# Transposing the hidden rows between an expert's two layers with VectorE's 32 by 32 blocks and a trip through memory

## The reference, cut to what matters

```python
for e in range(E):                                   # E = 8
    for k in range(2):
        mask = top2[:, k] == e
        h = np.maximum(x[mask] @ w1[e], 0.0)         # [n, 512] @ [512, 1024], ReLU
        out[mask] += top2_w[mask, k, None] * (h @ w2[e])   # [n, 1024] @ [1024, 512]
```

## Time and profile before

| what | value |
|---|---|
| median of 3 runs | 1077.09 us (1076.47 to 1077.72) |
| the profiled execution | 1075.87 us, its span 1074.0 us |
| granted TensorE clock | 0.999 of full speed |
| TensorE busy | 1062.9 us, 99% |
| VectorE busy | 586.2 us, 55% |
| ScalarE busy | 328.3 us, 31% |
| GpSimd busy | 386.9 us, 36% |
| experts' stage | from about 560 us to the end |

### The profile page before, as it was taken

The page is one execution under the profiler, slowest core; times in us unless marked ns, Lnnn a source line. Parts: engine busy times, 40 slices in busy tenths (PEclk is TensorE's granted clock), DMA queues, the critical chain, the costliest instruction groups (busy, mean ns, idle before and its releaser), DMA issues.

```text
span 1074.0 us, 20103 instructions
## 1 busy us (share of the span) xinstructions
PE 1062.9 (99%) x6053; PEld 932.2 (87%) x6054; DVE 586.2 (55%) x1226; ACT 328.3 (31%) x724; POOL 386.9 (36%) x358
## 2 busy tenths in 40 slices
PE   8999999999999999999999999999999999999997
PEld 7888999999999999999988888888888888888886
DVE  6887344363463463453447775555565555556553
ACT  7986222342432432432352111020303020110231
POOL 4667990030030030210184424060706042240586
PEclk9999999999999999999999999999999999999999
DMA  8985525411311312211175435271626244332676
GB/s 230 283 269 183 161 88 190 125 60 30 118 60 30 117 59 34 93 60 30 47 238 166 140 97 158 44 207 41 195 49 173 71 131 118 88 92 49 171 243 222
DMA packets 199635, 133.18 MB, mean 124 GB/s; under 512 B 128753, under 2 KB 161409, under 8 KB 199585
## 3 DMA queue, kind: packets, MB, share of 16 engines
q1 hardware_dynamic: 177728, 75.14, 25.9%
q10 hardware_dynamic: 16032, 38.47, 11.1%
q0 software_dynamic: 5824, 18.95, 5.1%
HBM read 85.87 MB, written 42.73 MB: 120 GB/s over the span
## 4 chain that ended last, share of the span: by engine, by line
PE 97%; DVE 1%; ACT 1%; issue 1%; DMA 0%; DVEq 0%; SPq 0%; ACTq 0%
PE bank L872 28%; PE bank L1040 22%; PE bank L1061 22%; PE bank L904 14%; PE bank L1074 3%; PE bank L816 2%; PE bank L843 2%; PE bank L826 1%; PE bank L810 1%; PE bank L957 1%; DMA k_sb<-in_kT 0%; ACT p_sb L1216 0%; PE bank L1139 0%; PE bank L885 0%; DVE xT L1234 0%
## 5 line engine op out<-in xcount | busy, mean ns | idle before, releaser
L872 PE MATMUL bank<-x_parts,mlp_weights 128*128 128x384 f32 x1704 | 309.4, 336 | 0.0
L872 PEld LDWEIGHTS bank<-x_parts,mlp_weights 128*128 128x128 f32 x1704 | 298.3, 188 | 5.3
L1040 PE MATMUL bank<-expert_parts,xT_high 128*128 (+1 forms) x688 | 216.7, 396 | 0.0
L1061 PE MATMUL bank<-expert_parts,hT_high 128*128 (+1 forms) x688 | 212.3, 390 | 1.4 <-DVE hT_low L1818 1.4
L731 POOL TENSOR_TENSOR expert_parts<-raw_expert_a,expert_parts 128x512 fp32r<-128x512 f32 x64 | 81.4, 1306 | 234.2 <-ACT expert_parts L1366 231.9
L904 PE MATMUL bank<-mlp_weights,hidden_parts 128*128 128x512 f32 x648 | 162.2, 395 | 0.0
L1061 PEld LDWEIGHTS bank<-expert_parts,hT_high 128*128 128x128 f32 x688 | 129.1, 188 | 28.6 <-issue 2.0
L1040 PEld LDWEIGHTS bank<-expert_parts,xT_high 128*128 128x128 f32 x688 | 125.8, 188 | 24.3 <-issue 0.4
L904 PEld LDWEIGHTS bank<-mlp_weights,hidden_parts 128*128 128x128 f32 x648 | 120.3, 188 | 23.3 <-issue 1.0
L1040 PE MATMUL bank<-expert_parts,xT_low 128*128 (+1 forms) x344 | 134.5, 391 | 0.0
L1061 PE MATMUL bank<-expert_parts,hT_low 128*128 (+1 forms) x344 | 134.3, 390 | 0.0
(11 more groups left out here) (220 smaller groups left out, 1229.6 us busy)
## 6 DMA issues: line engine op xcount, KB each, us to landing
raw_expert_a<-in_w ACTq DMA_DIRECT2D x32, 512.0 KB, 4.6
raw_expert_b<-in_w ACTq DMA_DIRECT2D x32, 512.0 KB, 4.0
x_row<-routed_rows SPq DMA_DIRECT2D x172, 64.0 KB, 2.6
expert_rows<-y_row SPq DMA_DIRECT2D x43, 256.0 KB, 2.0
expert_rows<-zeros SPq DMA_DIRECT2D x4, 2304.0 KB, 11.8
v_sb<-in_v SPq DMA_DIRECT2D x32, 256.0 KB, 4.0
q_sb<-in_qT SPq DMA_DIRECT2D x15, 288.0 KB, 3.7
k_sb<-in_kT SPq DMA_DIRECT2D x15, 288.0 KB, 4.3
```

The lines of the kernel that those rows point to most:

```text
L872: last = nc.tensor.matmul(bank[:, 0:CHUNK], w_sb[:, i, wp, at:at + P], xp[:, par, part, k, :], start=n == 0, stop=n == 3 * KB - 1)
L1040: last = nc.tensor.matmul(ps[half][:, 0:512], (xTh, xTl)[xp][:, buf, k, :], ew_sb[:, bass.ds(slot, 1), wp, k * F2 + half * 512:k * F2 + ha ...
L1061: last = nc.tensor.matmul(y_bank(t)[:, 0:D], (hTh, hTl)[hp][:, f, :], ew_sb[:, bass.ds(slot, 1), 2 + wp, f * D:(f + 1) * D].rearrange("p a ...
```

## The change

For tiles 4 to 41 TensorE no longer transposes the hidden rows. VectorE transposes the 32 by 32 blocks of each half on the way out of PSUM into a new buffer `hB`, without the ReLU (`dve_turn`). SyncE stores `hB` (512 KB) to a scratch tensor in memory, waits for it, and loads it back in four DMAs, one for each quarter of the partitions, into `relu`, so that each block is in its transposed place (`move_hidden`). VectorE then takes the ReLU and splits into `hTh` and `hTl`: per half one `tensor_scalar` and four `scalar_tensor_tensor` of 128 columns (`dve_hidden`). Tiles 0 to 3 and 42 go through TensorE as before; the last tile is reordered, with its transposes between the two halves of the second layer of tile 41, and its result goes to bank 4.

```diff
--- before.py
+++ after.py
@@ -55,6 +55,7 @@
     xT_dram = nc.dram_tensor("xT_scratch", [PAIRS, P, TOKENS], F32).ap()
     xs_dram = nc.dram_tensor("routed_rows", [E * STRIDE, D], F32).ap()
     ye_dram = nc.dram_tensor("expert_rows", [ETILES * P, D], F32).ap()
+    hs_dram = nc.dram_tensor("hidden_by_blocks", [P, F2], F32).ap()
 
 
     ROW = 512
@@ -90,6 +91,9 @@
     raw_mlp = at("raw_mlp", [P, 2, COLS], F32, STAGE_OFF)
     raw_exp_a = at("raw_expert_a", [P, 2, 1024], F32, STAGE_OFF)
     y_sb = at("y_sb", [P, CHUNK_TILES, D], F32, STAGE_OFF + 2 * 4096)
+
+    hB = at("hidden_blocks", [P, F2], F32, STAGE_OFF + 2 * 4096)
+    assert F2 <= CHUNK_TILES * D
 
     yT_sb = at("yT_sb", [P, CHUNK_TILES, KB, P], F32, STAGE_OFF + D * 4)
     assert D * 4 + CHUNK_TILES * KB * P * 4 <= 2 * 4096
@@ -346,7 +350,10 @@
         hTh_done = sem("hTh_done")
         hTl_done = sem("hTl_done")
         tile_done = sem("tile_done")
-        second_tile_half_done = sem("second_tile_half_done")
+
+        half_done = sem("half_done")
+        hidden_out = sem("hidden_out")
+        hidden_in = sem("hidden_in")
         y_row_done = sem("y_row_done")
         y_row_out = sem("y_row_out")
         ye_zeroed = sem("ye_zeroed")
@@ -402,6 +409,9 @@
 
 
 
+        FIRST_TURNED = 4
+
+
         TO_T, TO_PV = 3, 4
 
 
@@ -587,12 +597,31 @@
             load_rows(3, 1)
             load_rows(4, 0)
             store_rows(1)
-            with sp.Fori(0, (ETILES - 5) // 2) as m:
+            load_rows(5, 1)
+            store_rows(2)
+            load_rows(6, 0)
+
+            def move_hidden(t):
+
+                sp.wait_ge(relu_done, 2 * t + 2)
+                sp.dma_start(hs_dram, hB[:]).then_inc(hidden_out, 16)
+                sp.wait_ge(hidden_out, 16 * (t + 1 - FIRST_TURNED))
+                blocks = hs_dram.rearrange("(s r) (h q n) -> q r h s n", s=BLOCKS, h=2, q=BLOCKS)
+                for q in range(BLOCKS):
+                    sp.dma_start(relu[q * BLOCK:(q + 1) * BLOCK, :].rearrange("r (h s n) -> r h s n", h=2, s=BLOCKS),
+                                 blocks[q]).then_inc(hidden_in, 16)
+
+            assert FIRST_TURNED == 4 and (ETILES - 3 - FIRST_TURNED) % 2 == 0
+            with sp.Fori(0, (ETILES - 3 - FIRST_TURNED) // 2) as m:
                 for a in range(2):
-                    load_rows(2 * m + (5 + a), (5 + a) % 2)
-                    store_rows(2 * m + (2 + a))
-            for t in range(ETILES - 3, ETILES):
-                store_rows(t)
+                    move_hidden(2 * m + (FIRST_TURNED + a))
+                    load_rows(2 * m + (FIRST_TURNED + 3 + a), (FIRST_TURNED + 3 + a) % 2)
+                    store_rows(2 * m + (FIRST_TURNED - 1 + a))
+            for t in range(ETILES - 3, ETILES - 1):
+                move_hidden(t)
+                store_rows(t - 1)
+            store_rows(ETILES - 2)
+            store_rows(ETILES - 1)
 
             sp.wait_ge(y_row_out, 16 * ONE + 16 * ETILES)
             sp.wait_ge(rows_out, 16 * (CHUNKS - 1 + CHUNK_TILES))
@@ -1045,12 +1074,12 @@
 
         def y_bank(t):
 
-            return ps[4] if isinstance(t, int) and t == 2 else ps[5]
+            return ps[4] if isinstance(t, int) and t in (2, ETILES - 1) else ps[5]
 
         def pe_down2(pe, t, slot, expert, halves=(0, 1)):
             if halves[0] == 0:
                 pe.wait_ge(expert_low, 16 * expert + 16)
-                if not (isinstance(t, int) and t in (0, 2)):
+                if not (isinstance(t, int) and t in (0, 2, ETILES - 1)):
 
                     pe.wait_ge(y_row_done, ONE + t)
             n = 3 * 4 * halves[0]
@@ -1062,7 +1091,7 @@
                                                 ew_sb[:, bass.ds(slot, 1), 2 + wp, f * D:(f + 1) * D].rearrange("p a n -> p (a n)"),
                                                 start=n == 0, stop=n == 3 * FB2 - 1)
                         n += 1
-            last.then_inc(tile_done if halves[-1] == 1 else second_tile_half_done, 1)
+            last.then_inc(tile_done if halves[-1] == 1 else half_done, 1)
 
         def pe_hT(pe, t):
             for b in range(2):
@@ -1111,10 +1140,8 @@
 
                 now = entries(t)
                 before = entries(t - 1)
-                pe_hT(pe, t - 1)
                 pe_up2(pe, t, buf, *now)
                 pe_down2(pe, t - 1, *before)
-                return now
             fourth = entries(3)
             pe_up2(pe, 3, 1, *fourth)
             fifth = entries(4)
@@ -1125,10 +1152,15 @@
             with pe.Fori(0, (ETILES - 7) // 2) as m:
                 tile(2 * m + 5, 1)
                 tile(2 * m + 6, 0)
-            tile(ETILES - 2, (ETILES - 2) % 2)
-            now = tile(ETILES - 1, (ETILES - 1) % 2)
-            pe_hT(pe, ETILES - 1)
-            pe_down2(pe, ETILES - 1, *now)
+            t = ETILES - 1
+            tile(t - 1, (t - 1) % 2)
+            now = entries(t)
+            before = entries(t - 1)
+            pe_up2(pe, t, t % 2, *now)
+            pe_down2(pe, t - 1, *before, (0,))
+            pe_hT(pe, t)
+            pe_down2(pe, t - 1, *before, (1,))
+            pe_down2(pe, t, *now)
 
         @block.tensor
         def _(pe):
@@ -1806,9 +1838,9 @@
 
         def dve_hT(dve, t, halves=(0, 1)):
             for b in halves:
-                dve.wait_ge(hT_done, 2 * t + b + 1)
-                if isinstance(t, int) and t == 2 and b == 0:
-                    dve.wait_ge(second_tile_half_done, 1)
+                dve.wait_ge(hT_done, 2 * min(t, FIRST_TURNED) + b + 1)
+                if isinstance(t, int) and t in (2, ETILES - 1) and b == 0:
+                    dve.wait_ge(half_done, 1 if t == 2 else 2)
                 elif not (isinstance(t, int) and t == 0):
 
                     dve.wait_ge(tile_done, t)
@@ -1822,11 +1854,38 @@
         def dve_relu(dve, t, halves=(0, 1)):
             for half in halves:
                 dve.wait_ge(up_done, 2 * t + half + 1)
-                if not (isinstance(t, int) and t == 0):
+                if isinstance(t, int) and 0 < t < FIRST_TURNED:
 
                     dve.wait_ge(hT_done, 2 * t - 1 + half)
+                elif isinstance(t, int) and t == ETILES - 1:
+
+                    dve.wait_ge(hTl_done, 2 * t)
                 nc.vector.tensor_scalar(relu[:, half * 512:half * 512 + 512], ps[half][:], 0.0, None, ALU.max
                                         ).then_inc(relu_done, 1)
+
+        def dve_turn(dve, t):
+
+            for half in range(2):
+                dve.wait_ge(up_done, 2 * t + half + 1)
+                nc.vector.transpose(hB[:, half * 512:half * 512 + 512].rearrange("p (q f c) -> p q f c", q=BLOCKS, c=BLOCK),
+                                    ps[half][:].rearrange("p (f q c) -> p q f c", q=BLOCKS, c=BLOCK)
+                                    ).then_inc(relu_done, 1)
+
+        def dve_hidden(dve, t):
+
+            dve.wait_ge(hidden_in, 16 * BLOCKS * (t + 1 - FIRST_TURNED))
+            dve.wait_ge(tile_done, t)
+            for b in range(2):
+                landed = relu[:, b * 512:b * 512 + 512].rearrange("p (s f c) -> p f s c", s=BLOCKS, c=BLOCK)
+                h = hTh[:, 4 * b:4 * b + 4, :].rearrange("p f (s c) -> p f s c", c=BLOCK)
+                nc.vector.tensor_scalar(h, landed, 0.0, None, ALU.max).then_inc(hTh_done, 1)
+                dve.wait_ge(hTh_done, 2 * t + b + 1)
+                low = hTl[:, 4 * b:4 * b + 4, :].rearrange("p f (s c) -> p f s c", c=BLOCK)
+                for s in range(BLOCKS):
+                    last = nc.vector.scalar_tensor_tensor(out=low[:, :, s], in0=landed[:, :, s], scalar=0.0,
+                                                          in1=h[:, :, s].bitcast(F32), op0=ALU.max,
+                                                          op1=ALU.subtract)
+                last.then_inc(hTl_done, 1)
 
         def dve_y(dve, t):
             dve.wait_ge(tile_done, t + 1)
@@ -1863,25 +1922,29 @@
             dve_xT(dve, 4, 0, 2)
             dve_relu(dve, 3)
             for t, extra in ((4, dve_places), (5, dve_combine)):
-                dve_hT(dve, t - 1)
-                dve_relu(dve, t)
+                if t == FIRST_TURNED:
+                    dve_hT(dve, t - 1)
+                else:
+                    dve_hidden(dve, t - 1)
+                dve_turn(dve, t)
                 dve_xT(dve, t + 1, (t + 1) % 2, (t + 1) // 2)
                 extra(dve, link)
                 dve_y(dve, t - 1)
 
             def tile(t, buf, earlier):
-                dve_hT(dve, t - 1)
-                dve_relu(dve, t)
+                dve_hidden(dve, t - 1)
+                dve_turn(dve, t)
                 dve_xT(dve, t + 1, buf, earlier)
                 dve_y(dve, t - 1)
             with dve.Fori(0, (ETILES - 7) // 2) as m:
                 tile(2 * m + 6, 1, m + 3)
                 tile(2 * m + 7, 0, m + 4)
             t = ETILES - 1
-            dve_hT(dve, t - 1)
+            dve_hidden(dve, t - 1)
             dve_relu(dve, t)
+            dve_hT(dve, t, (0,))
```

(2 more changed lines are left out.)

## The result

The changed kernel takes 1173.07 us (median of 4 runs, 1169.91 to 1175.42) against 1077.40 for the kernel before on the same chip: ratio 1.088, 95% interval 1.087 to 1.090. It is slower by 95.7 us. The profiled execution took 1169.91 us, its span is 1168.1.

The account below looks back on a forecast made before the run. TensorE alone was taken to set the 11.80 us tile, with an 11.9 us loop through memory and VectorE in its place; -2.3 + 5 + 65 + 12.5 = +80 on 1075.87 gave 1156 us, range 1072 to 1195.

Parts of the forecast that it names:

- rival A: Experts' stage: hidden-row loop is about 11.9 us and GpSimd takes turns with VectorE; 1156 us, own range 1120 to 1190; 46%.
- Quiet tiles: Tiles without expert weight loading: trip through memory and VectorE takes 11.9 us against 11.8 before, about +5 over 38 tiles.
- Rival D: Short loop hidden behind TensorE's 10.9 us, and VectorE keeps the port shared with GpSimd; 1067 us, down to 1041; 15%.
- Turns with GpSimd: In six weight-loading bursts, VectorE's short two-input instructions of hidden(t) wait for GpSimd's subtractions: 8.8 us a burst.
- the case that I priced at 2.5 and left out: VectorE's SBUF-to-SBUF copies in hidden(t) are blocked by GpSimd too: 2.5 us more, not counted in the sum.
- Rival B: Loop about 11.9 us, but VectorE keeps the port over its four short instructions, waiting once a half; 1111 us; 22%.
- Transfers in a burst: Stores and loads of hidden rows land later beside the expert weight loads: 2.0 us in each of six bursts.
- the first trip's loads meet one weight piece: A burst's first hidden-row loads meet just one weight piece; a full meeting was put at 1.4 us for loads.
- the next, delayed, what is left of them: A burst's second hidden-row trip comes late and meets only the remaining weight loads; both trips together 2.0 us a burst.
- The end: Last five tiles: the trip is slowed beside the gathers and GpSimd's adds, 2.5 us each, 12.5 in all.
- The last tile: Reordered tile 42: TensorE's hole of 2.27 us, waiting for VectorE to split the transposed halves, goes; -2.3 us.
- SyncE's queue: The x rows and y store standing behind the waiting move are issued within 9.7 us, under 11.9: costs nothing.

## Why the prediction was right

Right: the sign, the size (1156 for 1173, within 1072 to 1195) and the mechanism, rival A. That the sum came within 14 us of its execution (1169.91) is in part luck, as its terms were off in both directions: quiet tiles came 16 us cheaper than forecast, bursts 18 dearer, the end 8 and the last tile 4.

- **Quiet tiles.** 11.9 was predicted, 11.46 measured. The store took 2.57 (2.9 in the sum), the three issue steps 1.95 (1.65; within the 1.2 to 2.2), the last landing 3.06 (2.5, and above its upper bound of 2.9), hidden(t) 2.54 (3.1, below its lower bound of 2.6), the turn 1.31 (1.33), and the gaps between engines 0.1 (0.44). What made hidden(t) short: 512 columns are copied from SBUF to SBUF in 0.43 us, 1.5 times the pace of line 1196 in the earlier trace rows. That is the Trainium skill's rule (VectorE: DVE Perf Modes, Mode 2×_2P), by which such a copy runs twice as fast; the trace agrees with it (from SBUF to PSUM the same columns take 0.69). The row is read rightly, but it doesn't stand for this copy; no run shows why line 1196 is slower. The Trainium skill's 2.0 us and bytes over 436 GB/s (DMA: Bandwidth & Descriptors, Anatomy of one DMA) made an estimate of 3.2 for the store, and the trace has 2.57; the section measured DMAs that GpSimd issues, and this one is SyncE's. In all -12.6 + 1.7 = -11 in place of +5: the loop is a little shorter than TensorE's old tile, and longer than its new one. Rival D asked for 10.9.
- **Turns with GpSimd.** 8.8 a burst was predicted with the copies not blocked; 10.3 read and 10.4 measured alone. The four short instructions of a half wait about as the step said (5.05 and 5.09 in place of 0.90 each, 8.3 more); the copies are blocked too, another 1.28 + 1.50 - 0.85 = 1.9. That is the case that I priced at 2.5 and left out. Rival B falls: VectorE does not keep the port between its instructions.
- **Transfers in a burst.** 2.0 was predicted; 13.9 - 10.3 = 3.6 is paid on top of the turns, and 6.8 to 8.3 without them. The term was too small in both of its steps. In "the first trip's loads meet one weight piece" the loads pay 2.1 on the mean, more than the 1.4 that I gave for a full meeting. In "the next, delayed, what is left of them" the store pays 1.7 on the mean, from nothing to 4.1.
- **The end.** 12.5 was predicted, for five tiles; 20.4 is measured, over four periods. Three pay 3.1 to 3.6 each, not 2.5, nearly all by the last load's landing (2.9 to 3.4 over 3.06). The last pays 10.2: its store 4.4, its load 4.1, and a copy held by GpSimd's additions 1.5.
- **The last tile.** -2.3 was predicted; TensorE's hole was not the only thing that ended there, and alone the new order gave +0.7 us. What lies outside the periods, where this term stands in the sum, is +1.4.
- **SyncE's queue** held nothing, as said: its store of y is out at 704.05 + 0.39, before the turn at 704.90. **TensorE's** part, "nothing, up to 0.3 a tile", was low: it idles 0.4 to 0.9 once per pass of two tiles, up to 0.45 a tile, hidden in the changed kernel and bare as soon as the loop is shorter.

Summed: -11 + 83 + 20.4 + 1.4 = 94, against -2.3 + 5 + 65 + 12.5 = 80.

## What to carry to other kernels

When work is moved off the engine that sets the time, add up the loop through the other engines' queues, with everything that stands in order in them, and compare it with the new time of that engine. If the two are near, give the trip slack (one more tile between producer and user) before making any part of it faster; then look at who waited behind the old bound, here the gathers of the end and a gap per pass of the loop.

## What the runs showed of the hardware that was not expected

- A short two-input instruction of VectorE on SBUF and GpSimd's subtraction alternate one by one: 1.26 us each for 128 columns that take 0.22 alone. Beside GpSimd's memset these short instructions are not held (a single record is 0.29 us at the median and 0.37 at most).
- Copies from SBUF to SBUF are held by both kinds of GpSimd's instructions: 0.43 us becomes 1.28 to 1.50 beside the subtractions and up to 0.88 beside a memset. The subtractions hold neither a copy from SBUF to PSUM (0.68 to 0.70 in all 76) nor a transpose from PSUM to SBUF (0.67 to 0.72 in all 76).
- TensorE idles 0.4 to 0.9 us once per pass of its own loop over two tiles, when no long wait covers it and the pass opens with a first layer. Twice as many tiles in a pass halve the number of gaps; wholly straight code left 4 of 19 and was no faster.
- Four DMAs issued one after another start 0.65 us apart (0.61 and 0.04); the 1.95 us of the three steps are a sixth of this loop's 11.46.
